# The first MLP's expanding product, by Strassen's scheme, with weights streamed from a scratch in DRAM

## The chip, the cores and the metric

One Trainium2 chip, of which this kernel uses one core. The time is device microseconds of one execution; the kernel before took 1018.35 us (median of two runs, 1016.62 to 1020.07). Engines are named as the profile names them: PE (TensorE, with PEld for its weight loads), DVE (VectorE), ACT (ScalarE), POOL (GpSimd) and SP (SyncE, which here only issues DMAs). Each runs its own list of instructions in order and waits for the others through semaphores.

## The reference, cut to what matters

```python
def _moe_ref(x, w_ch1, w_ch2):          # x: (4, 768, 512), the attention's output
    X = np.fft.fft(np.fft.fft(x, axis=1), axis=2)
    u = x + np.real(X)                  # "mix" is the second term
    un = (u - mean(u)) / np.sqrt(var(u) + 1e-06)
    ch = np.maximum(un @ w_ch1, 0.0) @ w_ch2      # 512 -> 2048 -> 512: the first MLP
    return u + ch
```

Ahead of it stands a windowed attention (8 heads of 64), behind it a second block (`_moe2_ref`): 512 -> 1024 with relu, a convolution of three taps along the sequence, a sigmoid gate, 1024 -> 512. All in float32.

## The kernel before, in words

**Precision.** The large products run in the one-pass float32 format of PE (`fp32r`). Each operand is kept as a high part, which is that rounding of it, and a low part, which is the rest; a product is three matmuls: low by high, high by low, high by high, added up in one PSUM bank.

**Three stages.** (1) `attention_and_fourier` handles the four batches of 768 tokens and leaves `mix` (the Fourier part) in a DRAM scratch. The order of its steps on each engine is written out by hand in the table `ORDER`: on PE the words `seq`, `dim` and `mix` are the two Fourier products and the turning of their result, on ACT `bh` and `mk` round or copy the results of `seq` and `mix`, on DVE `bl` and `cm` make the low parts and the combinations. Words `mlp0`, `mlp1`, ... in the last batch call the first steps of the next stage (`first_tensor`, `first_scalar`, ...), so that the two stages overlap. (2) `channel_mlp` is the first MLP. (3) `gated_conv` is the second block.

**The first MLP.** It works on half batches of 384 tokens (8 of them, g), and on 16 tiles of 128 hidden channels (m). For each pair (g, m), `expand` (L807) makes 384 tokens by 128 hidden channels from 4 chunks of 128 inputs: 12 matmuls of 384 columns. ACT (L722) takes relu and rounds (`h_hi`), DVE (L783) makes the low part (`h_lo`), and `contract` (L822) multiplies it with the second weight: 9 matmuls of 512 columns into three PSUM banks that add up over all 16 m. `expand` of m+1 stands before `contract` of m, so PE has work while ACT and DVE prepare h. In between DVE adds `mix` to u (L738), takes the statistics (L742, L747), normalises the next half (L771), PE turns it (L796, 4 transposes for 128 tokens) and ACT and DVE split it (L716, L777).

**Weights.** All 16 tiles of both weights stay in SBUF, 128x1024 numbers each: SP loads a tile (L686, three buffers, 512 KB), ACT rounds it (L708), DVE makes the low part (L729). This happens once, in the first half batch. `mix_in` for three tiles of tokens comes in one DMA of 768 KB (L679).

## Time and profile before

| | |
|---|---|
| median of two runs | 1018.35 us |
| the profiled execution | 1019.49 us, of which the span of the trace is 1017.4 us |
| granted PE clock, mean | 0.988 |
| busy: PE, DVE, ACT, POOL | 983.8, 433.2, 296.5, 175.3 us |
| matmuls | 6360 |
| first MLP's steady stretch | about 205 to 741 us |
| second block | 741 to 1017 us |

Busy times are sums over one engine; PE's matmuls overlap in the trace (a matmul's end is modelled), so what a matmul costs is read from the distance between starts, not from its own duration. A clock of 1.00 is 2.4 GHz and 0.50 is 1.2 GHz.

### The profile page before, as it was taken

To read this page: it belongs to the slowest core of one execution; us is meant where nothing else is said; L and a number is where in the kernel's file an instruction comes from. 1 tells how busy PE (TensorE), PEld (TensorE's weight loads), DVE (VectorE), ACT (ScalarE), POOL (GpSimd) and SP (SyncE) were. 2 spreads that over 40 slices of the span, in tenths; PEclk is the share of its full clock that TensorE was granted. 3 is DMA by queue.
4 is the path that set the end of the run, shared out by engine and by line. 5 is a ranking of instruction groups with operands and counts; after the bars stand their busy time and mean duration, and the time that the engine had idled before them with its cause. 6 is when DMAs were issued, how large, how long until landed. Compare 5 with 4: busy or idle time off the path is not lost.

```text
span 1017.4 us, 15409 instructions
## 1 busy us (share of the span) xinstructions
PE 983.8 (97%) x6360; PEld 885.5 (87%) x6360; DVE 433.2 (43%) x670; ACT 296.5 (29%) x535; POOL 175.3 (17%) x167
## 2 busy tenths in 40 slices
PE   4998997999999999999999999999999999999998
...
GB/s 337 397 220 312 310 155 229 203 146 43 93 1 1 93 1 36 58 1 93 0 0 93 0 31 62 1 129 91 42 93 1 65 60 1 124 0 41 21 1 63
DMA packets 41401, 92.73 MB, mean 91 GB/s; under 512 B 6912, under 2 KB 7040, under 8 KB 41088
## 3 DMA queue, kind: packets, MB, share of 16 engines
...
q0 software_dynamic: 576, 3.55, 0.9%
q8 instruction: 42, 0.69, 0.3%
...
## 4 chain that ended last, share of the span: by engine, by line
PE 92%; DMA 3%; SPq 1%; DVE 1%; issue 1%; POOL 1%; ACT 1%; ACTq 0%; POOLq 0%
PE ps L807 26%; PE ps L822 26%; PE ps L1171 13%; PE ps L1181 13%; PE ps L542 7%; DMA k_win<-in_k 3%; PE ps L506 2%; PE ps L533 2%; PE ps L1154 1%; PE ps L796 1%; PE ps L516 1%; SPq L249 1%; PE ps L598 1%; SPq L259 0%; SPq L245 0%
## 5 line engine op out<-in xcount | busy, mean ns | idle before, releaser
L807 PE MATMUL ps<-un_hi,w 128*128 128x384 f32 x1024 | 285.8, 339 | 1.6 <-ACT mix_sb L401 1.6
L822 PE MATMUL ps<-w,h_hi 128*128 128x512 f32 x768 | 241.0, 395 | 0.0
L807 PEld LDWEIGHTS ps<-un_hi,w 128*128 128x128 f32 x1024 | 187.2, 188 | 6.2 <-ACT mix_sb L401 1.8
L783 DVE SCALAR_TENSOR_TENSOR h_lo<-ps,h_hi 128x384 fp32r<-128x384 f32 x128 | 71.2, 556 | 280.1 <-ACT h_hi L722 280.1
L722 ACT ACTIVATE h_hi<-ps 128x384 fp32r<-128x384 f32 x128 | 62.9, 492 | 375.6 <-PE ps L807 375.6
L807 PE MATMUL ps<-un_lo,w 128*128 128x384 f32 x512 | 171.8, 336 | 0.0
L822 PEld LDWEIGHTS ps<-w,h_hi 128*128 128x128 f32 x768 | 144.0, 187 | 27.6
L822 PE MATMUL ps<-w,h_lo 128*128 128x512 f32 x384 | 149.4, 389 | 0.9 <-DVE h_lo L783 0.9
L1171 PE MATMUL ps<-y_hi,v 128*128 128x384 f32 x512 | 130.7, 334 | 0.8 <-issue 0.8
L1181 PE MATMUL ps<-v,g_hi 128*128 128x512 f32 x384 | 118.8, 391 | 0.0
L1136 DVE SCALAR_TENSOR_TENSOR conv<-h_pad,taps,conv 128x768 f32<-128x768 f32 x64 | 100.5, 1570 | 2.3
L1237 POOL TENSOR_TENSOR g_lo<-conv,g_hi 128x768 fp32r<-128x768 f32 x32 | 68.7, 2153 | 186.8 <-ACT g_hi L1105 186.8
L807 PEld LDWEIGHTS ps<-un_lo,w 128*128 128x128 f32 x512 | 96.2, 188 | 4.2
L1231 POOL MEMSET h_pad<- 128x6 f32 x1 | 0.1, 108 | 575.3 <-PE ps L822 575.3
L1171 PEld LDWEIGHTS ps<-y_hi,v 128*128 128x128 f32 x512 | 92.4, 188 | 1.3 <-issue 1.2
L1171 PE MATMUL ps<-y_lo,v 128*128 128x384 f32 x256 | 85.5, 334 | 0.0
L1181 PEld LDWEIGHTS ps<-v,g_hi 128*128 128x128 f32 x384 | 72.2, 188 | 14.8
L822 PEld LDWEIGHTS ps<-w,h_lo 128*128 128x128 f32 x384 | 72.2, 188 | 12.7 <-DVE h_lo L783 1.2
L1181 PE MATMUL ps<-v,g_lo 128*128 128x512 f32 x192 | 76.5, 398 | 0.0
L1171 PEld LDWEIGHTS ps<-y_lo,v 128*128 128x128 f32 x256 | 48.1, 188 | 0.1
L1124 DVE TENSOR_TENSOR y_lo<-ps,y_hi 128x512 fp32r<-128x512 f32 x24 | 16.6, 692 | 69.0 <-ACT y_hi L1086 69.0
L506 PE MATMUL ps<-k_win,q_sb 128*32 128x128 f32 x768 | 30.2, 305 | 14.5 <-DMA k_win<-in_k 14.5
...
## 6 DMA issues: line engine op xcount, KB each, us to landing
...
k_win<-in_k SPq DMA_DIRECT2D x48, 256.0 KB, 5.2
...
q_sb<-in_q SPq DMA_DIRECT2D x24, 256.0 KB, 4.7
mix_scratch<-mix_sb ACTq DMA_DIRECT2D x24, 256.0 KB, 6.2
u_sb<-x_scratch SPq DMA_DIRECT2D x8, 768.0 KB, 4.6
mix_in<-mix_scratch SPq DMA_DIRECT2D x8, 768.0 KB, 6.2
y_scratch<-u_sb SPq DMA_DIRECT2D x8, 768.0 KB, 3.6
```

Of the source, the lines that this page charges most:

```text
L506: last = nc.tensor.matmul(out, q_sb[:, n % NB, a, toks], k_win[:, n % NB, :, a, c, :], start=True, stop=True)
L533: last = nc.tensor.matmul(out, p_sb[:, t % 2, a, toks], v_win[:, n % NB, :, c, a, :], start=True, stop=True)
L542: last = nc.tensor.matmul(out, lhs, rhs, start=(n == 0), stop=(n == 3 * len(terms) - 1))
L722: nc.scalar.activation(h_hi[:, m % 2, :], ps[:, BH + m % 2, 0:HALF], ACT.Relu).then_inc(h_hi_ready, 1)
L783: nc.vector.scalar_tensor_tensor(out=h_lo[:, m % 2, :], in0=ps[:, BH + m % 2, 0:HALF], scalar=0.0, in1=h_hi[:, m % 2, :].bitcast(F32), op0 ...
L807: last = nc.tensor.matmul(ps[:, BH + m % 2, 0:HALF], w[:, cols], x[:, par, c, :], start=(k == 0), stop=(k == 3 * ND - 1))
L822: last = nc.tensor.matmul(ps[:, BACC[s], :], h[:, m % 2, cols], w, start=(m == 0 and j == 0), stop=(m == M1T - 1 and j == 2))
L1124: nc.vector.tensor_tensor(y_lo[:, :, cols], ps[:, BT, :].rearrange("p (c n) -> p c n", c=ND), y_hi[:, :, cols].bitcast(F32), ALU.subtract) ...
L1136: nc.vector.scalar_tensor_tensor(out=c, in0=h[:, j:S + j], scalar=taps[:, m, j:j + 1], in1=c, op0=ALU.mult, op1=ALU.add).then_inc(tap_done ...
L1171: last = nc.tensor.matmul(ps[:, BH[m % 2] + half, 0:HALF], w[:, cols], y[:, c, toks], start=(k == 0), stop=(k == 3 * ND - 1))
L1181: last = nc.tensor.matmul(ps[:, BACC[t], :], g[:, m, cols], w, start=(m == 0 and j == 0), stop=(m == M2T - 1 and j == 2))
L1237: nc.gpsimd.tensor_tensor(g_lo[:, m, :], conv[:, m % 3, :], g_hi[:, m, :].bitcast(F32), ALU.subtract).then_inc(g_lo_ready, 1)
```

## The change

The first MLP's `expand` takes a whole batch at once (768 tokens as two halves of 384), and a pair of hidden tiles (256 channels), as a product of 2 by 2 blocks: inputs 256 + 256, channels 128 + 128, tokens 384 + 384. Strassen's scheme (in Winograd's form) computes it with 7 products of blocks in place of 8, and 7 additions on the results; both operands need 4 sums of blocks each. There are 8 pairs for a batch (`PAIRS`) and 32 in all.

- **PE.** A pair is 7 products of 6 matmuls of 384 columns, each product in a PSUM bank of its own. Four pairs are expanded one after the other, and then their 8 hidden tiles are contracted for all 768 tokens into 6 banks (a group g, two for each batch): 18 matmuls of 512 columns for a tile.
- **ACT, DVE.** The results of a pair are added up in SBUF (`keep_first`, `combine`, `complete`: one copy on ACT, 7 additions on DVE), and relu and low part are then taken from SBUF, four times for a pair. After each group DVE adds the six accumulators to u (`add_up`).
- **Operands.** `upper`, `lower`, `upper_sums` and `lower_sums` make the 4 blocks and the 4 sums of the tokens (128x1024 numbers are rounded for 128 columns of the sums); POOL makes the 4 sums of a pair's weight blocks (`sums`, 128x256 numbers each), ACT and DVE round 128x7x256 numbers for a pair (`weights1`).
- **Weights.** They no longer fit in SBUF: 3 buffers for pairs (14,336 bytes a partition) and 4 for tiles of the second weight. In the first batch SP loads them raw, and stores high and low parts to a scratch in DRAM; from the second batch on POOL loads these from there (`stream_w1`, `stream_w2`).
- **Loads of mix** come one tile of tokens at a time through two buffers, each waiting for an addition on DVE (`load_mix`).
- **Order.** The words `mlpN` in the table stand for other steps and at other places; the loops over batches are written out. The second block differs in where its weights lie and when they are loaded.

```diff
+PAIRS, GROUP = 8, 8
...
+        "mix2.1 mix2.2 mix2.3 mix2.4 mix2.5 seq3.0 seq3.1 seq3.2 seq3.3 mlp0 seq3.4 seq3.5 mlp1 dim3.0 mlp2 "
+        "seq3.6 seq3.7 mlp3 dim3.1 mix3.0 mix3.1 mix3.2 mix3.3 mix3.4 mix3.5 mlp4 "
...
+        "mirror2.1 mk2.0 mk2.1 split3.5 mk2.2 mk2.3 mk2.4 mk2.5 bh3.0 mlp0 bh3.1 bh3.2 mlp1 mlp2 bh3.3 bh3.4 "
+        "mlp3 mlp4 bh3.5 mlp5 mlp6 mlp7 qs3.0 bh3.6 mirror3.0 bh3.7 mlp10 qs3.1 mirror3.1 mk3.0 mk3.1 mk3.2 "
+        "mk3.3 mk3.4 mk3.5 mlp8 mlp11 mlp9 "
...
+        "mlp0 mlp1 bl3.0 mlp2 mlp3 bl3.1 bl3.2 mlp4 mlp5 bl3.3 bl3.4 mlp6 mlp7 mlp8 bl3.5 mlp9 mlp10 mlp11 "
+        "mlp12 cm3.0 bl3.6 bl3.7 mlp15 cm3.1 mlp13 mlp16 mlp14 "
...
+        "lower3.3 fold3.5 lower3.4 lower3.5 mlp0 mlp1 mlp2 "
...
+    PRODUCTS = ((A11, B11), (S2, T2), (A12, B21), (S1, T1), (S3, T3), (S4, B22), (A22, T4))
+    P1, P6, P2, P5, P7, P3, P4 = range(7)
...
+    def load_mix(eng, b, s):
+        n = b * TILES + s
+        if n >= 2:
+            eng.wait_ge(u_ready, n - 1)
+        eng.dma_start(mix_in[:, s % 2], mix_dram[b, s]).then_inc(ld_mix[s % 2], 16)
+    def load_raw1(sp, n):
+        if n >= 3:
+            sp.wait_ge(product_done, 7 * (n - 2))
+            sp.wait_ge(st_w1[n % 3], 16 * (n // 3))
+        sp.dma_start(w1_raw[n % 3][:, A11:A12 + 1:A12 - A11, 1], w[2 * n][:, 0].rearrange("p (k c) -> p k c", k=2)
+                     ).then_inc(ld_raw1[n % 3], 16)
+        sp.dma_start(w1_raw[n % 3][:, S1:A22 + 1:A22 - S1, 1], w[2 * n + 1][:, 0].rearrange("p (k c) -> p k c", k=2)
+                     ).then_inc(ld_raw1[n % 3], 16)
...
+    def load_raw2(sp, j):
+        if j >= 4:
+            await_contracted(sp, j - 4)
+            sp.wait_ge(st_w2[j % 4], 16 * (j // 4))
+        sp.dma_start(w2_raw[j % 4][:, 1], w[j][:, 1]).then_inc(ld_raw2[j % 4], 16)
...
+    def store_w2(sp, j):
+        sp.wait_ge(w2_ready, j + 1)
+        sp.dma_start(w2_dram[j], raw(w2[j % 4][:])).then_inc(st_w2[j % 4], 16)
+    def stream_w1(pool, n):
+        pool.wait_ge(product_done, 7 * (n - 2))
+        if n < 2 * PAIRS:
+            pool.wait_ge(st_w1[(n - PAIRS) % 3], 16 * ((n - PAIRS) // 3 + 1))
+            pool.wait_ge(st_w1[n % 3], 16 * len([m for m in range(PAIRS) if m % 3 == n % 3]))
+        pool.dma_start(w1[n % 3][:], w1_dram[n % PAIRS]).then_inc(ld_w1[n % 3], 16)
...
+        sp.wait_ge(core.folded, 3 * TILES)
+        for i in range(FOLDS):
+            sp.wait_ge(core.st_x[i], 16 * (B - 1))
+        load_u(sp, 0)
...
+        for s in range(2):
+            load_mix(sp, 0, s)
...
+        load_raw1(sp, 0)
+        for s in range(2, TILES):
+            load_mix(sp, 0, s)
+        sp.wait_ge(core.seq_done, 8 * B)
+        for n in (1, 2):
+            load_raw1(sp, n)
...
+            nc.gpsimd.tensor_tensor(part(S3), part(A11), part(S1), ALU.subtract).then_inc(s_added, 1)
+            pool.wait_ge(s_added, 3 * n + 1)
+            nc.gpsimd.tensor_tensor(part(S1), part(S1), part(A22), ALU.add).then_inc(s_added, 1)
+            pool.wait_ge(s_added, 3 * n + 2)
+            nc.gpsimd.tensor_tensor(part(S2), part(S1), part(A11), ALU.subtract).then_inc(s_added, 1)
+            pool.wait_ge(s_added, 3 * n + 3)
+            nc.gpsimd.tensor_tensor(part(S4), part(A12), part(S2), ALU.subtract).then_inc(s_ready, 1)
...
+        def weights1(n):
+            act.wait_ge(s_ready, n + 1)
+            nc.scalar.activation(w1[n % 3][:, :, 0], w1_raw[n % 3][:, :, 1], ACT.Copy).then_inc(w1_hi_ready, 1)
...
+            for m, half, sums in ((2 * n, 0, 2), (2 * n, 1, 5), (2 * n + 1, 0, 6), (2 * n + 1, 1, 7)):
+                act.wait_ge(summed, 7 * n + sums)
+                nc.scalar.activation(hidden(m, half, 0), raw_hidden(m, half), ACT.Relu).then_inc(relu_done, 1)
...
+        def weights1(n):
+            dve.wait_ge(w1_hi_ready, n + 1)
+            nc.vector.tensor_tensor(w1[n % 3][:, :, 1], w1_raw[n % 3][:, :, 1], raw(w1[n % 3][:, :, 0]), ALU.subtract
+                                    ).then_inc(w1_ready, 1)
...
+        def plus(n, out, a, i):
+            dve.wait_ge(product_done, 7 * n + i + 1)
+            nc.vector.tensor_tensor(out, a, result(n, i), ALU.add).then_inc(summed, 1)
...
+        def combine(n):
+            c11, c12, c21, c22 = (raw_hidden(2 * n + r, half) for r in range(2) for half in range(2))
+            dve.wait_ge(copied, n + 1)
+            plus(n, c21, c12, P6)
+            plus(n, c11, c12, P2)
+            dve.wait_ge(summed, 7 * n + 2)
+            plus(n, c12, c21, P5)
+            plus(n, c22, c21, P7)
+            low_part(n, 2 * n, 0, 1)
...
+            c11, c12, c21, c22 = (raw_hidden(2 * n + r, half) for r in range(2) for half in range(2))
+            dve.wait_ge(summed, 7 * n + 4)
+            plus(n, c12, c12, P3)
+            plus(n, c21, c22, P4)
+            dve.wait_ge(summed, 7 * n + 6)
+            plus(n, c22, c22, P5)
+            low_part(n, 2 * n, 1, 2)
+            low_part(n, 2 * n + 1, 0, 3)
+            low_part(n, 2 * n + 1, 1, 4)
...
-        def expand(m, par):
...
-            for c in range(ND):
-                cols = slice(c * P, (c + 1) * P)
-                for w, x in ((w1_lo, un_hi), (w1_hi, un_lo), (w1_hi, un_hi)):
-                    last = nc.tensor.matmul(ps[:, BH + m % 2, 0:HALF], w[:, cols], x[:, par, c, :],
...
+        def expand(n):
...
+            if n < PAIRS:
+                pe.wait_ge(w1_ready, n + 1)
+            else:
+                pe.wait_ge(ld_w1[n % 3], streamed(n))
+            for i, (weight, tokens) in enumerate(PRODUCTS):
...
+                    elif i == P5:
+                        pe.wait_ge(summed, 7 * n)
...
+                for c in range(2):
+                    w_hi, w_lo = (w1[n % 3][:, weight, j, c * P:(c + 1) * P] for j in range(2))
+                    t_hi, t_lo = x_hi[:, tokens, c, :], x_lo[:, tokens, c, :]
+                    for a, b in ((w_lo, t_hi), (w_hi, t_lo), (w_hi, t_hi)):
+                        last = nc.tensor.matmul(result(n, i), a, b, start=(k == 0), stop=(k == 5))
+                        k += 1
+                last.then_inc(product_done, 1)
...
+            j, n = g * GROUP + m, 4 * g + m // 2
+            if j < M1T:
+                pe.wait_ge(w2_ready, j + 1)
...
+            for t in range(TILES):
...
+                        pe.wait_ge(summed, 7 * (4 * g + 3) + t)
+                    elif t == P5:
+                        pe.wait_ge(summed, 7 * (4 * g + 4))
...
+                for i, (part, weight) in enumerate(((1, 0), (0, 1), (0, 0))):
+                    last = nc.tensor.matmul(ps[:, t, :], h[:, m, part, cols], w2[j % 4][:, weight],
...
+        if k == 0:
...
+        elif k < 7:
+            (upper if k % 2 else upper_sums)(0, (k - 1) // 2)
+        elif k < 10:
+            weights1(k - 7)
+        else:
+            keep_first(k - 10)
+            rectify(k - 10)
...
+        if k < 2:
+            for s in range(3 * k, 3 * k + 3):
+                add(0, s)
+            for s in range(3 * k, 3 * k + 3):
+                stats(0, s)
+            if k == 1:
+                variance(0)
+        elif k == 2:
             inverse_root(0)
...
+        elif k in (3, 5, 8):
+            normalise(0, (3, 5, 8).index(k))
+        elif k in (4, 7, 10):
+            lower(0, (4, 7, 10).index(k))
+        elif k in (6, 9, 11):
+            lower_sums(0, (6, 9, 11).index(k))
+        elif k < 15:
+            weights1(k - 12)
+        else:
+            combine(k - 15)
+            complete(k - 15)
...
+        if k < 3:
+            turn(0, k)
+        else:
+            expand(k - 3)
...
+            for g in range(2 * B):
+                b, second = divmod(g, 2)
+                for p in range(4):
+                    n = 4 * g + p
+                    if n < PAIRS:
+                        store_w1(sp, n)
+                    if n + 3 < PAIRS:
+                        load_raw1(sp, n + 3)
+                    if g == 0 and p >= 2:
+                        for j in (2 * p - 4, 2 * p - 3):
+                            store_w2(sp, j)
...
+                if not second and b + 1 < B:
+                    load_u(sp, b + 1)
+                    for s in range(2):
+                        load_mix(sp, b + 1, s)
...
+                for m in range(GROUP):
+                    j = g * GROUP + m + 4
+                    if 4 < j <= M1T:
+                        store_w2(sp, j - 1)
+                    if j < M1T:
+                        load_raw2(sp, j)
+                    if not second and b + 1 < B and 1 <= m <= 4:
+                        load_mix(sp, b + 1, m + 1)
...
+            for g in range(1, 2 * B):
+                for p in range(4):
+                    if PAIRS <= 4 * g + p + 3 < B * PAIRS:
+                        stream_w1(pool, 4 * g + p + 3)
+                for m in range(GROUP):
+                    if M1T <= g * GROUP + m + 4 < B * M1T:
+                        stream_w2(pool, g * GROUP + m + 4)
...
+            for g in range(2 * B):
+                b, second = divmod(g, 2)
+                for p in range(4):
+                    n = 4 * g + p
+                    if n >= 2:
+                        combine(n)
+                        if 3 <= n + 1 < PAIRS and n + 1 not in (5, 6):
+                            weights1(n + 1)
+                        complete(n)
...
+                for m in range(GROUP):
+                    j = g * GROUP + m + 3
+                    if 4 <= j < M1T:
+                        weights2(j)
+                    if g == 0 and m in (0, 3):
+                        weights1(5 + m // 3)
+                    if not second and b + 1 < B and m < TILES:
+                        add(b + 1, m)
+                        stats(b + 1, m)
...
+                for t in range(TILES):
+                    add_up(g, t)
...
+            for g in range(2 * B):
+                b, second = divmod(g, 2)
+                for p in range(4):
+                    if 4 * g + p >= 2:
+                        expand(4 * g + p)
+                for m in range(GROUP):
                     contract(g, m)
...
+                    if second and b + 1 < B and m in (0, 2, 4):
+                        turn(b + 1, m // 2)
...
+        sp.wait_ge(core.product_done, 7 * B * PAIRS)
...
-            pe.wait_ge(core.y_ready, 2 * B * SUBS)
+            pe.wait_ge(core.y_ready, (2 * B - 1) * TILES + 4)
```

**What the order shows, ACT, end of the Fourier stage.** L401 to L409 copy `mix` (the words `mk3.*`) and L393 stores it; L813 rounds a pair's weights, L843 and L848 are `keep_first` and `rectify`. In the kernel before a tile's rounding (L708) stands among the `bh` steps; after it, on ACT:

```order
L409 ACTIVATE mix_sb<-ps 128x2
L393 DMA mix_scratch<-mix_sb 128x512
L813 ACTIVATE w_1_64<-w_1_raw 128x7x256
L843 ACTIVATE h_raw<-ps 128x384
L848 ACTIVATE h<-h_raw 128x384 x4
L813 ACTIVATE w_2_62<-w_2_raw 128x7x256
```

The second pair's weights are rounded behind the last copy of `mix`, and the third pair's behind the relus of the second.

**DVE, the first steps of the MLP.** Before (u and `mix` added, statistics, then the first `b_lo` of the last batch, L465):

```order
L738 TENSOR_TENSOR u_sb<-u_sb,mix_in 128x512 x3
L742 BN_STATS bn<-u_sb 128x6 x3
L747 BN_AGGR mv<-bn 128x2 x3
L749 TENSOR_SCALAR root<-mv 128x3
L465 TENSOR_TENSOR b_lo<-ps,b_hi 128x386
```

and of the change (the same `b_lo` is L473):

```order
L871 BN_STATS bn<-u_51 128x6 x3
L867 TENSOR_TENSOR u_51<-u_51,mix_in 128x512 x3
L871 BN_STATS bn<-u_51 128x6 x3
L876 BN_AGGR mv<-bn 128x2 x6
L878 TENSOR_SCALAR root<-mv 128x6
L473 TENSOR_TENSOR b_lo<-ps,b_hi 128x386
```

Six tiles of tokens instead of three now stand ahead of `b_lo`, and further down the rounding of the first pair (L855) stands ahead of the combination `cm3.0` (L483, L484):

```order
L928 TENSOR_TENSOR x_lo<-x_lo_raw,x_hi 128x8x128
L855 TENSOR_TENSOR w_0_60<-w_0_raw,w_0_60 128x7x256
L483 TENSOR_TENSOR m_all<-ps,q_sin 128x385
L484 TENSOR_TENSOR m_all<-ps,q_sin 128x385
L473 TENSOR_TENSOR b_lo<-ps,b_hi 128x386 x2
L935 TENSOR_TENSOR h_raw<-h_raw,ps 128x384 x4
L939 SCALAR_TENSOR_TENSOR h<-h_raw,h 128x384
```

**SP, the first contraction.** `w_0_raw` to `w_3_raw` are here the four buffers of the second weight, `w_scratch` the DRAM scratch:

```order
L738 DMA w_0_raw<-in_moe_w 128x512 [waits st_w2_0,contracted]
L746 DMA w_scratch<-w_0_68 128x1024 [waits w2_ready]
L738 DMA w_1_raw<-in_moe_w 128x512 [waits st_w2_1,contracted]
L721 DMA mix_in<-mix_scratch 128x512 [waits u_ready]
L746 DMA w_scratch<-w_1_70 128x1024 [waits w2_ready]
L738 DMA w_2_raw<-in_moe_w 128x512 [waits st_w2_2,contracted]
```

Each raw load of a tile stands behind the store of the tile before it, which waits until ACT and DVE have rounded that one.

## Rows read from the trace of the kernel before

**Rows 1.** The page, part 2: PE busy in tenths, 40 slices.
```profile
PE   4998997999999999999999999999999999999998
```
**Rows 2.** PE's timeline, steady MLP; start us, us, engine, line, form.
```profile
651.12 0.33 PE L807 MATMUL ps<-un_hi,w 128*128 128x384 f32 x1
...
653.22 0.39 PE L822 MATMUL ps<-w,h_lo 128*128 128x512 f32 x1
...
655.30 0.60 PE L796 MATMUL ps<-ident_sb,un 128*128 128x128 f32 x4
```
**Rows 3.** The page, part 5: busy, mean ns | idle before, releaser.
```profile
L807 PE MATMUL ps<-un_hi,w 128*128 128x384 f32 x1024 | 285.8, 339 | 1.6 <-ACT mix_sb L401 1.6
...
L783 DVE SCALAR_TENSOR_TENSOR h_lo<-ps,h_hi 128x384 fp32r<-128x384 f32 x128 | 71.2, 556 | 280.1 <-ACT h_hi L722 280.1
L722 ACT ACTIVATE h_hi<-ps 128x384 fp32r<-128x384 f32 x128 | 62.9, 492 | 375.6 <-PE ps L807 375.6
```
**Rows 4.** Windows: length, PE PEld DVE ACT POOL, PEclk, DMA share, GB/s.
```profile
165.00:741.00 576.00, 572.10 (x2934) 519.21 (x2934) 190.80 (x361) 118.90 (x231) 0.40 (x2) 1.00 0.17 58
...
40.00:45.00 5.00, 5.00 (x56) 4.52 (x56) 2.27 (x5) 2.60 (x5) 4.92 (x7) 1.00 1.04 410
```
**Rows 5.** PE's timeline, the last batch's first Fourier products.
```profile
165.17 0.66 PE L542 MATMUL ps<-seq_hi,z_lo 128*128 128x386 f32 x1 [0.83 <-ACT mix_sb L406]
...
168.20 0.44 PE L542 MATMUL ps<-seq_hi,z_lo 128*128 128x386 f32 x1
...
171.45 0.34 PE L542 MATMUL ps<-seq_hi,z_lo 128*128 128x386 f32 x1
```
**Rows 6.** DVE's timeline, the MLP's first steps.
```profile
163.48 2.97 DVE L738 TENSOR_TENSOR u_sb<-u_sb,mix_in 128x512 f32<-128x512 f32 x3 [5.16 <-DMA mix_in<-mix_scratch]
166.37 1.87 DVE L742 BATCH_NORM_STATS2 bn<-u_sb 128x6 f32<-128x512 f32 x3
...
168.62 0.17 DVE L749 TENSOR_SCALAR root<-mv 128x3 f32<-128x3 f32 x1
```
**Rows 7.** DMA issues: KB each, median us to landing.
```profile
mix_in<-mix_scratch SPq DMA_DIRECT2D x8, 768.0 KB, 6.2
...
out<-o_sb SPq DMA_DIRECT2D x24, 256.0 KB, 2.0
```
**Rows 8.** The line of the tile w_raw: landings of its 512 KB loads.
```profile
DMA to landing us min/median/max: 3.2/3.7/8.2
```
**Rows 9.** Groups by form: busy us, mean ns | idle before.
```profile
L1142 DVE TENSOR_TENSOR conv<-h_pad,conv 128x768 f32<-128x768 f32 x32 | 30.3, 948 | 0.2
...
L729 DVE TENSOR_TENSOR w<-w_raw,w 128x1024 fp32r<-128x1024 f32 x16 | 19.5, 1218 | 11.7 <-ACT w L708 11.7
...
L310 POOL TENSOR_TENSOR z_raw<-sums 128x256 f32<-128x256 f32 x24 | 17.5, 731 | 1.9
...
L708 ACT ACTIVATE w<-w_raw 128x1024 fp32r<-128x1024 f32 x16 | 16.8, 1052 | 0.5 <-ACT mix_sb L401 0.5
...
L777 DVE TENSOR_TENSOR un_lo<-ps,un_hi 128x512 fp32r<-128x512 f32 x24 | 16.6, 692 | 43.4 <-ACT un_hi L716 43.4
...
L357 ACT ACTIVATE z_hi<-z_raw 128x512 fp32r<-128x512 f32 x24 | 15.1, 628 | 13.6 <-POOL z_raw L311 10.9 <-ACT mix_sb L401 1.2 <-ACT mix_sb L396 0.9
...
L716 ACT ACTIVATE un_hi<-ps 128x512 fp32r<-128x512 f32 x24 | 14.4, 598 | 42.5 <-PE ps L796 42.5
```
**Rows 10.** ACT's timeline, copies of mix.
```profile
195.09 0.39 ACT L393 ACTIVATE mix_sb<-ps 128x256 f32<-128x256 f32 x1 [0.47 <-PE ps L598]
...
196.29 0.39 ACT L393 ACTIVATE mix_sb<-ps 128x256 f32<-128x256 f32 x1 [0.47 <-ACT mix_sb L396]
```
**Rows 11.** DVE's timeline, second block: first without, then beside POOL's work.
```profile
747.42 2.07 DVE L1136 SCALAR_TENSOR_TENSOR conv<-h_pad,taps,conv 128x768 f32<-128x768 f32 x2
...
760.59 3.55 DVE L1136 SCALAR_TENSOR_TENSOR conv<-h_pad,taps,conv 128x768 f32<-128x768 f32 x2
```

More of the change, by code:

```diff
@@ new lines, in raw, with streamed, turn_bank, hidden @@
+    def raw(t):
+        return t.bitcast(F32)
+    def streamed(n):
+        return 16 * len([m for m in range(PAIRS, n + 1) if m % 3 == n % 3])
+    def turn_bank(b, r):
+        return (2 if b == 0 else 6) + r
+    def hidden(m, half, part):
+        return h[:, m % GROUP, part, half * HALF:(half + 1) * HALF]
+    def raw_hidden(m, half):
+        return h_raw[:, m % GROUP, 1, half * HALF:(half + 1) * HALF]
+    def bank(n, i):
+        return i % 5 if n < 2 else i
+    def result(n, i):
+        return ps[:, bank(n, i), 0:HALF]
@@ L920, in _ @@
+        @block.gpsimd
+        def _(pool):
+            sums = on_gpsimd(pool)
+            for n in range(3, PAIRS):
+                sums(n)
+            for g in range(1, 2 * B):
[5 more added lines that the diff above has]
+                        stream_w2(pool, g * GROUP + m + 4)
         @block.scalar
```

641 lines of the change are left out of this document (314 added, 327 removed), and 8 rows, old and new, of the table ORDER.

## The prediction

> **What bounds the kernel now.** I read the busy shares first: PE is busy in nearly every slice of the MLP [rows 1], so what a matmul costs decides. Its own duration (339 ns, [rows 3]) overlaps with its neighbour's and can't be used. The timeline can: from 651.12 to 653.22 us stand the 12 matmuls of one `expand`, from there to 655.30 the 9 of one `contract` [rows 2]. That is 0.175 us for a matmul of 384 columns and 0.231 us for one of 512. DVE and ACT wait for PE in this stage (280 and 376 us of idle time before their h steps, [rows 3]), DMA is nearly idle, and PE lost only 576.0 - 572.1 = 3.9 us between 165 and 741 us [rows 4]. So fewer matmuls give their whole price, as long as nothing else makes PE wait. Everything up to 165 us and the second block I take as unchanged.
>
> **What is removed.** For a pair of hidden tiles and a batch, 48 matmuls of 384 columns become 42: 6 x 32 pairs = 192, at 0.175 us **33.6 us**. The 1152 matmuls of `contract` and the 96 turnings stay. The Trainium skill (TensorE: Matmul & The Clock Gate, "Back-to-back issue gap") gives N/2.4 + 2.5 ns, 162.5 ns here; by that the gain would be 31.2 us. The row decides.
>
> **Steady state after.** A pair takes PE 42 x 0.175 = 7.34 us. DVE has 7 additions from PSUM and 4 low parts from SBUF. An addition is like L783, 0.56 us [rows 3]. The low part now reads SBUF twice: two of L1136 on 768 numbers took 2.07 us [rows 11], a number costs (1218 - 948)/256 = 1.055 ns [rows 9], so 384 numbers take 1.03 - 0.41 = 0.62 us. Together 6.4 us, under 7.34. ACT has one copy and four relus of 0.5 us [rows 3]. A group is 4 x 7.34 + 8 x 4.15 = 62.6 us, in which 4 x 1.84 + 8 x 0.52 = 11.5 MB come from the scratch, 185 GB/s where 410 were moved [rows 4]. One block of 1.84 MB needs 4.5 us by that rate and about 2 us to start, and has two pairs' time, 14.7 us. So from the second batch on I cost the streaming and the sums at nothing; their cover is the 0.9 us a pair by which PE is longer than DVE.
>
> **What is added: the start.** The first batch pays for the rounding and for steps put in front of others. Prices: rounding a pair's 1792 numbers takes DVE 1.218 + 768 x 1.055 ns = 2.03 us, and ACT 1.052 + 768 x (1052 - 628)/512 ns = 1.69 us [rows 9]. POOL's four sums of 256 numbers take 4 x 0.73 = 2.9 us [rows 9]. Splitting 128 columns of tokens: ACT 0.6 + 3 x 0.27 = 1.4 us, DVE 1.8 us for the four sums and 1.0 us for two low parts, from 0.69 us for 512 numbers and 0.42 for 256 [rows 9]; ACT and DVE 1.0 and 1.2 us for 1024 numbers of the sums; normalising two tiles 1.0, a turning and its signal 1.0. A load of 256 KB lands in 2.0 us at the least [rows 7], and in less than the 3.7 us (3.2 at best) of 512 KB [rows 8]. I take 2.6 alone and 3.2 right behind a store of 512 KB.
>
> Walking the orders with these, PE waits:
> - a. **`seq3.3`, 6.9 us.** It needs the first `b_lo`, which now stands behind six tiles' additions and statistics. Before, three tiles came by one DMA and the variance was done at 168.8 [rows 6]. Now the third to sixth tile are each asked for only after an addition. First addition 164 (POOL's work slows it, as the 2.97 us for three show, [rows 6]); third 168; statistics 1.87; fourth 171; its buffer's load lands 173.9; last addition 174.6; statistics, variance 177.8; `b_lo` 178.3. PE arrives at 171.4 [rows 5].
> - b. **turning 1 and `dim3.0`, 8.2 us.** In line on DVE and ACT: turn 1.0, split 1.4 + 2.8, normalise 1.0, the same again, `b_lo` 0.5, 12.9 us; PE has 4.8 us of its own there.
> - c. **`seq3.7`, 7.7 us.** `dim3.0` 3.3, turn 1.0, split 1.4 + 1.8, sums 1.0, rounding of pair 0 1.7 + 2.0, `cm3.0` 1.0, 13.2 us; PE has 5.7.
> - d. **`mix3`, 3.9 us:** 1.8 behind pair 0's additions, 2.1 because ACT needs 1.20 us for a copy [rows 10].
> - e. **pair 1, 6.9 us:** three copies of `mix` are left, then 1.7 + 2.0.
> - f. **pair 2, 5.4 us:** its rounding stands behind pair 1's last additions and relu (1.7), then 1.7 + 2.0.
> - g. **pair 3, the first `contract` and pair 7, 1.2 us each:** 2.0 us of rounding stand between a pair's additions.
> - h. **pair 4, 11.6 us.** In the first contraction a raw tile is asked for only once the one before is rounded and its store issued: 0.3 + 3.2 + ACT 0.6 + DVE 0.65 + 0.4 = 5.2 us, where PE needs 4.15 us for a tile. Seven tiles stand ahead of DVE's `add_up`, without which PE may not reuse the banks; the chain also starts 2 us late, behind the next batch's loads of u, and pair 6's rounding lies in it.
> - i. **turnings of the later batches, 4.3 us** together.
>
> Sum 58.5 us. After a gap PE is slow too: from 165.17 to 168.20 nine matmuls took 3.03 us, the next nine to 171.45 two times 1.6 [rows 5], as if the clock were 1.2 GHz for 3 us. I charge 1.45 us for each of b, c, e, f and h, 7.2 us.
>
> DVE's work from two SBUF operands collides with POOL's sums: two L1136 took 3.55 us in place of 2.07 beside POOL [rows 11]. The Trainium skill (SBUF — State Buffer, "Who interferes with whom") makes this a lock: whoever starts first holds the shared ports for its whole instruction. By that a rounding waits for one sum at most, 0.7 us; were the ports shared by time, its 2.0 us would become about 3.4. POOL is rarely at work when DVE rounds, so I add nothing and leave 0 to 5 us to the range.
>
> **Sum.** 1019.5 (the profiled execution) - 33.6 - 3.9 (the old waits, counted anew) + 58.5 + 7.2 = 1047.7; the median lies 1.1 under the profiled execution, so **1046 us**.
>
> **Rivals.** About 2% (20 us) is what a measurement tells from no change.
> - *As summed* (60%): slower, 1034 to 1060. The waits a to f rest on the written order and on durations of rows; landings of 2.0 or 3.7 us move a and h by -10 to +8.
> - *The second weight keeps pace* (25%), the case on the other side: if a load lands in 2.1 us or less, h's period is 4.1 us, PE's own. Then h and its slow clock go, 13 us: 1033, not slower by the 2%. For it: 2.0 us for 256 KB [rows 7]. Against: that is a store, alone on its queue, and here a store of 512 KB goes ahead.
> - *DVE becomes the bound* (11%): 6.4 us leave 0.9 a pair. Each addition waits for a product or for its forerunner; with 0.15 us more for each of the 11, or one lock of 1.5 us a pair from POOL's DMAs, a pair takes 8.1 us, and 28 pairs 0.8 us more each: 1068.
> - *The gain stands* (4%): DVE and ACT run so far ahead that a to h are the old waits: 1018.4 - 33.6 = 985. Only a misread order would give it.
> - That the change doesn't save the matmuls is excluded: its list holds 1344 of 384 columns against 1536.
>
> Faster by over 2%: 3%. Within 2%: the second case and the low end of the first, 30%. Slower: 67%. The range for 8 in 10 is 1030 to 1066, which takes in the second case and nearly reaches the third.
>
> **What would show it.** The new profile should have PE's slices lower between 170 and 310 us only, full ones after; gaps before the first `b_lo`'s reader, `cm3.0`'s reader, pairs 1, 2 and 4, of 5 to 12 us, their releasers DVE; the start of the second block 25 to 30 us later than 741. A gap before pair 4 under 3 us means the second case. Waits of PE for DVE's additions or for a streamed block in each later group mean the third. I am wrong altogether if the MLP's first contraction starts before 240 us.

## The result and the profile after

The changed kernel took 1058.06 us (median of two runs, 1055.83 and 1060.29), the kernel before 1018.35: a ratio of 1.039, 95% interval 1.0269 to 1.0511. In a later set of runs on one chip (e11 below) it was 1060.38 against 1017.0, ratio 1.041, 1.0384 to 1.0436. So it is slower by 4%, at the upper end of the range forecast (1030 to 1066). The profiled execution took 1055.83 us, span 1054.0.

The page of the changed kernel, part 2, busy share in 40 slices (of 26.35 us each), answers to [rows 1]:

```profile
PE   5999986567859989999999999999999999999998
...
PEclk9899997678988989999999999999999999999999
```

The 7th to 12th slice, 158 to 316 us, are low, and the clock with them; the 15th has an 8; from the 16th on every slice is full, as before. What the slices hold is in the waits, TensorE's alone, from 160 to 800 us (line waiting, what it waited for: sum in us, times, longest):

```profile
PE ps L1017 <- DVE w L855: 15.1, 4, 7.3
PE ps L550 <- DVE b_lo L473: 13.1, 2, 7.4
PE ps L1017 <- DVE u L966: 12.1, 1, 12.1
PE ps L979 <- DVE un L902: 7.9, 5, 3.8
PE ps L550 <- DVE m_all L484: 7.4, 1, 7.4
PE ps L1041 <- DVE w L860: 4.6, 4, 2.1
PE ps L606 <- DVE m_all L484: 2.0, 1, 2.0
PE ps L1041 <- DVE h_raw L935: 1.1, 1, 1.1
```

They add up to 63.3 us in 19 waits, all on VectorE's results. What the clock does behind a wait stands in the timeline of TensorE, here at pair 1 and pair 2 (columns as in [rows 2]; a bracket gives the wait before the instruction and what ended it):

```profile
233.20 0.69 PE L1017 MATMUL ps<-x_hi,w 128*128 128x384 f32 x1 [7.26 <-DVE w L855]
233.69 0.53 PE L1017 MATMUL ps<-x_lo,w 128*128 128x384 f32 x1
234.01 0.84 PE L1017 MATMUL ps<-x_hi,w 128*128 128x384 f32 x2
...
238.49 0.40 PE L1017 MATMUL ps<-x_lo,w 128*128 128x384 f32 x1
238.72 0.52 PE L1017 MATMUL ps<-x_hi,w 128*128 128x384 f32 x2
...
242.95 0.34 PE L1017 MATMUL ps<-x_hi,w 128*128 128x384 f32 x1
249.29 0.69 PE L1017 MATMUL ps<-x_hi,w 128*128 128x384 f32 x1 [6.00 <-DVE w L855]
```

Behind the wait a matmul follows the other by 0.32 us, from 238.7 us on by 0.176: some 16 matmuls lost 0.145 us each. The granted clock is 1.2 GHz in the first part and 2.4 in the second.

The steady part is as forecast. Two windows (columns as in [rows 4]), 100 us with most of a group, and one pair of the third batch:

```profile
520.00:620.00 100.00, 99.48 (x517) 92.27 (x516) 63.92 (x126) 20.16 (x41) 9.53 (x19) 1.00 0.69 241
...
542.34:549.72 7.38, 7.38 (x44) 7.38 (x43) 5.67 (x12) 2.48 (x5) 0.53 (x1) 1.00 0.76 279
```

A pair takes TensorE 7.38 us (42 matmuls by 0.1757; the sum had 7.34 instead of the old 8.40), VectorE 5.67.

**One stretch to compare by.** The attention part in front has waits for transfers that differ from run to run. So kernels are compared below by S: the time from the last weight load of the attention's scores (L514) to the first weight load of the second block's products (L1388), each read from one profiled execution. For the changed kernel these are the last number of the first row and the first of the second:

```profile
L514 PEld LDWEIGHTS ps<-k_win,q_sb x768: 105/110/178, 7.0 to 136.3; 128*32 128x32 f32 x192
...
L1388 PEld LDWEIGHTS ps<-y_hi,v x512: 187/188/188, 777.9 to 1017.7; 128*128 128x128 f32 x171
```

S is 641.6 us; before it was 741.3 - 142.7 = 598.6. The change costs 43.0 us there, while the span grew by 36.6: in this profile the attention part was 6.4 us shorter, and e11 shows that this is scatter.

| kernel | time, us | ratio to before (95%) | S, us |
|---|---|---|---|
| before | 1018.35 | 1 | 598.6 |
| changed | 1058.06 | 1.039 (1.027 to 1.051) | 641.6 |
| e11, the same again | 1060.38 | 1.041 (1.038 to 1.044) | 640.6 |
| e1, load ahead of store | 1038.78 | 1.021 (1.018 to 1.024) | 622.3 |
| e2, pairs 1 and 2 rounded early | 1053.21 | 1.035 (1.031 to 1.039) | 636.9 |
| e5, e2 and early store of pair 0 | 1047.89 | 1.029 (1.027 to 1.032) | 629.8 |
| e3, waits filled | 1048.22 | 1.029 (1.026 to 1.033) | 633.0 |
| e4, four cures | 1027.38 | 1.009 (1.006 to 1.011) | 608.5 |
| e6, eight cures | 1015.26 | 0.998 (0.996 to 0.9995) | 596.8 |
| e9, e6 with two places mended | 1010.42 | 0.992 (0.990 to 0.995) | 589.5 |
| e10, e9 with one wait filled | 1009.32 | 0.992 (0.990 to 0.995) | 591.6 |
| e7, two low parts twice | 1063.07 | 1.045 (1.042 to 1.047) | 642.4 |
| e8, four low parts twice | 1064.85 | 1.046 (1.043 to 1.048) | 648.5 |

The kernel before took 1017.5 beside e1 to e4, 1018.2 beside e5 to e8, 1017.0 beside e9 to e11. The letters a to i of the waits are those of the prediction.

### The profile page after: what moved, and what is told of

It is laid out like the page before. It is cut to its first block, busy times and chain, and to the rows that moved or that the text cites. A ratio compares the mean times of both kernels' runs of the same rounds, so it can differ in the third digit from the quotient of the medians.

```text
span 1054.0 us, 15426 instructions
## 1 busy us (share of the span) xinstructions
PE 964.6 (92%) x6168; PEld 866.9 (82%) x6168; DVE 597.1 (57%) x962; ACT 335.2 (32%) x607; POOL 238.6 (23%) x271
## 4 chain that ended last, share of the span: by engine, by line
PE 80%; DMA 9%; DVE 6%; ACT 2%; SPq 1%; issue 1%; POOL 0%; ACTq 0%; DVEq 0%; POOLq 0%
PE ps L1017 22%; PE ps L1041 20%; PE ps L1388 13%; PE ps L1398 12%; PE ps L550 6%; DMA w_raw<-in_moe_w 4%; PE ps L541 2%; DMA k_win<-in_k 2%; PE ps L514 2%; DMA mix_in<-mix_scratch 1%; DMA v_win<-in_v 1%; PE ps L979 1%; DVE h L939 1%; PE ps L1371 1%; PE ps L524 1%
## 5 line engine op out<-in xcount | busy, mean ns | idle before, releaser
L1041 PE MATMUL ps<-w,h 128*128 128x512 f32 x1152 | 270.3, 394 | 5.6 <-DVE w L860 4.6
L1017 PE MATMUL ps<-x_hi,w 128*128 128x384 f32 x896 | 239.0, 346 | 27.2 <-DVE w L855 15.1
L1041 PEld LDWEIGHTS ps<-w,h 128*128 128x128 f32 x1152 | 216.3, 189 | 51.7 <-DVE w L860 6.3
L1017 PEld LDWEIGHTS ps<-x_hi,w 128*128 128x128 f32 x896 | 167.9, 194 | 29.1 <-DVE w L855 16.3
L935 DVE TENSOR_TENSOR h_raw<-h_raw,ps 128x384 f32<-128x384 f32 x224 | 123.2, 553 | 74.5 <-PE ps L1017 68.3
L1017 PE MATMUL ps<-x_lo,w 128*128 128x384 f32 x448 | 154.1, 344 | 0.0
L1388 PE MATMUL ps<-y_hi,v 128*128 128x384 f32 x512 | 130.6, 334 | 0.0
L848 ACT ACTIVATE h<-h_raw 128x384 fp32r<-128x384 f32 x128 | 67.1, 526 | 164.2 <-DVE h_raw L935 162.0
L1388 PEld LDWEIGHTS ps<-y_hi,v 128*128 128x128 f32 x512 | 92.5, 188 | 0.2
L1017 PEld LDWEIGHTS ps<-x_lo,w 128*128 128x128 f32 x448 | 86.8, 194 | 0.2
L1388 PE MATMUL ps<-y_lo,v 128*128 128x384 f32 x256 | 85.6, 334 | 0.0
L939 DVE SCALAR_TENSOR_TENSOR h<-h_raw,h 128x384 fp32r<-128x384 f32 x128 | 68.4, 575 | 0.0
L966 DVE TENSOR_TENSOR u<-ps,u 128x512 f32<-128x512 f32 x48 | 31.9, 689 | 63.4 <-PE ps L1041 63.4
L843 ACT ACTIVATE h_raw<-ps 128x384 f32<-128x384 f32 x32 | 15.3, 478 | 139.5 <-PE ps L1017 139.5
L550 PE MATMUL ps<-seq_hi,z_lo 128*128 128x386 f32 x96 | 37.5, 391 | 15.2 <-DVE m_all L484 7.4
```

What stands on the lines that cost most here:

```text
L550: last = nc.tensor.matmul(out, lhs, rhs, start=(n == 0), stop=(n == 3 * len(terms) - 1))
L848: nc.scalar.activation(hidden(m, half, 0), raw_hidden(m, half), ACT.Relu).then_inc(relu_done, 1)
L935: nc.vector.tensor_tensor(out, a, result(n, i), ALU.add).then_inc(summed, 1)
L939: nc.vector.scalar_tensor_tensor(out=hidden(m, half, 1), in0=raw_hidden(m, half), scalar=0.0, in1=raw(hidden(m, half, 0)), op0=ALU.max, op ...
L966: nc.vector.tensor_tensor(u_sb[b % 2][:, t, :], ps[:, t, :], u_sb[b % 2][:, t, :], ALU.add).then_inc(y_ready, 1)
L1017: last = nc.tensor.matmul(result(n, i), a, b, start=(k == 0), stop=(k == 5))
```

## The experiments

**e11: is the shorter attention part the change's?**

> The changed kernel once more, in ten runs beside the kernel before, for a narrower ratio. If the five microseconds by which the attention part was shorter in its profile (its last scores at 136.7 us against 143.1) belong to the change, this profile shows them again; if they are scatter of the transfers there, the last scores end anywhere from 136 to 144 us, as in e1 to e8, and the median is 1055 to 1062.

```profile
L514 PEld LDWEIGHTS ps<-k_win,q_sb x768: 106/110/178, 6.9 to 144.3; 128*32 128x32 f32 x192
...
L1388 PEld LDWEIGHTS ps<-y_hi,v x512: 186/188/188, 784.9 to 1024.6; 128*128 128x128 f32 x171
```

The last scores of the same kernel now begin at 144.3 us instead of 136.3, and S agrees to 1 us. In all runs they lie between 136.3 and 144.3. It is scatter, and S is the number to read. Single waits scatter too: in e11 the later turning waits 3.1 us instead of 3.8 and the longest wait of the turning of mix is 2.8 instead of 2.0, so differences of that size between two profiles say nothing.

**e1: the second weight's serial chain (wait h).** Only the order of SyncE's issues in the contraction:

```diff
+                    if j < M1T:
+                        load_raw2(sp, j)
                     if 4 < j <= M1T:
                         store_w2(sp, j - 1)
-                    if j < M1T:
-                        load_raw2(sp, j)
```

> Only the order of SyncE's issues in the contraction of the first batch is changed: a raw tile of the second weight is asked for before the store of the one ahead of it, not behind it. Theory 'serial chain' (landing, two roundings and the store's signal in line, 5.2 us a tile where TensorE needs 4.15): the load then waits only for a free buffer, four tiles ahead of its use, so the three waits in the first contraction (0.84, 0.75, 0.93 us), most of the 12.1 us before pair 4 and the 3.8 us before a turning at 379 us go, and with them 4.5 us of slow clock: 22 us less, 1036 us; about 1 us is left before pair 4. Rival 'traffic' (the loads land late because stores, x and the second weight share the queues, whoever asks first): landings become longer by as much as they are asked earlier, and the time stays within 5 us of 1058. Rival 'DVE is late anyway': pair 4 keeps a wait of 5 us or more for the additions, and the time is 1045 or more.

First the chain in the changed kernel; the timelines of SyncE, ScalarE and VectorE in the first contraction:

```profile
291.82 0.32 SPq L746 DMA_DIRECT2D w_scratch<-w  x1
292.24 0.38 SPq L738 DMA_DIRECT2D w_raw<-in_moe_w  x1
...
295.56 0.63 ACT L817 ACTIVATE w<-w_raw 128x512 fp32r<-128x512 f32 x1 [4.50 <-DMA w_raw<-in_moe_w]
...
296.23 0.69 DVE L860 TENSOR_TENSOR w<-w_raw,w 128x512 fp32r<-128x512 f32 x1 [3.10 <-ACT w L817]
...
296.95 0.32 SPq L746 DMA_DIRECT2D w_scratch<-w  x1
...
317.32 0.69 DVE L860 TENSOR_TENSOR w<-w_raw,w 128x512 fp32r<-128x512 f32 x1 [4.28 <-ACT w L817]
317.93 3.67 DVE L966 TENSOR_TENSOR u<-ps,u 128x512 f32<-128x512 f32 x6
```

Asked at 292.24, on ScalarE at 295.56 (3.3 us), rounded by 296.9, and only then the next store and load: 5.13 us from store to store. The whole period from store to store is 5.0 to 5.6 us in this contraction. VectorE comes to the six `add_up` (L966) at 317.9, though TensorE had ended at 306.7. Behind the edit, TensorE's waits on these two lines in e1:

```profile
PE ps L1041 <- DVE w L860: 2.1, 1, 2.1
PE ps L1017 <- DVE u L966: 2.0, 1, 2.0
```

4.1 us are left of 16.7, and the 3.8 us before a turning at 379 us, of the same chain, are gone. S fell by 19.3 us, and the time by as much, of the 22 forecast: the chain was the cause. The rival "traffic" wanted landings longer by as much as they are asked for earlier; the median landing of the 256 KB loads went from 3.5 to 3.8 us.

**e2 and e5: the place of a rounding in the list (waits e and f).** e2 moves the rounding of pairs 1 and 2 (ScalarE's step 10 has pair 1's between its relus):

```diff
-... bh3.7 mlp10 qs3.1 mirror3.1 mk3.0 ... mk3.5 mlp8 mlp11 mlp9
+... bh3.7 mlp10 qs3.1 mlp9 mirror3.1 mk3.0 ... mk3.5 mlp11
-... mlp15 cm3.1 mlp13 mlp16 mlp14
+... mlp15 cm3.1 mlp13 mlp14 mlp16
```

> Only the place of the rounding of pairs 1 and 2 is changed: ScalarE rounds pair 1 between the relus of pair 0 and pair 2 ahead of the Fourier mirror, VectorE both right behind the Fourier combination and ahead of pair 1's additions. Theory 'written order' (waits e and f are the place of these two steps in the lists, the data being there since 218 us): the 7.3 us before pair 1 and the 6.0 us before pair 2 go, and 4 us of slow clock with them: 17 us less, 1041 us, with up to 2 us given back because the copies of the mix stand behind a rounding. Rival 'shared ports' (rounding is late because GpSimd's sums run beside it): VectorE's 2.03 us for a rounding become 3 us or more and pair 2 still waits over 3 us. Rival 'passed on': pair 3 and the first contraction inherit the wait, and the time is above 1050.

Both waits are gone, but S fell by 4.7 us only, not 17. Of the three theories "passed on" was right, and the trace of e2 shows where to; SyncE, GpSimd, VectorE and TensorE in order of time:

```profile
232.11 0.46 SPq L742 DMA_DIRECT2D w_scratch<-w  x1
241.79 0.38 SPq L728 DMA_DIRECT2D w_raw<-in_moe_w  x1
...
245.82 0.72 POOL L800 TENSOR_TENSOR w_raw<-w_raw 128x256 f32<-128x256 f32 x1 [23.22 <-DMA w_raw<-in_moe_w]
...
251.59 2.02 DVE L855 TENSOR_TENSOR w<-w_raw,w 128x1792 fp32r<-128x1792 f32 x1
...
253.67 0.69 PE L1017 MATMUL ps<-x_hi,w 128*128 128x384 f32 x1 [9.61 <-DVE w L855]
```

Pair 3 takes pair 0's buffer. The store of pair 0 is issued at 232.1 and has to land (9.7 us) before raw pair 3 is asked for; with landing, sums and roundings TensorE has it 21.6 us after the store. In the changed kernel pair 1 and 2 wait so long that this is hidden. So e5 adds, in SyncE's list ahead of its wait for the turned mix:

```diff
         for n in (1, 2):
             load_raw1(sp, n)
+        store_w1(sp, 0)
+        load_raw1(sp, 3)
```

> The kernel of e2, and the store of the rounded pair 0 and the load of raw pair 3 are issued by SyncE ahead of its wait for the turned mix (pair 0 is rounded at 204 us, its store was issued at 227 to 228). Theory 'passed on to the buffer': in e2 pair 3 waited 9.6 us because it takes the buffer of pair 0, whose 1.8 MB store had to land first, and the load, GpSimd's four sums and two roundings (some 11 us) come behind it; with the store 12 us or more earlier this wait falls under 2 us, its slow clock goes, and the 17 us forecast for e2 are there: 1041 us. Rival 'traffic' (the load of raw pair 3 lands late for whatever reason): pair 3 keeps over 5 us and the time stays at 1050.

```profile
215.92 0.47 SPq L742 DMA_DIRECT2D w_scratch<-w  x1
...
224.65 0.37 SPq L728 DMA_DIRECT2D w_raw<-in_moe_w  x1
```

Pair 3 waits 0.95 us now, S is 629.8: 11.8 us less than the changed kernel, of 17. Part of the rest was passed on once more, to what had been just in time: the fifth tile of the second weight waits 4.4 us instead of 2.1, and the first contraction 2.1 instead of 1.1. The turning of mix (3.7 instead of 2.0) and a later turning (5.1 instead of 3.8) are longer too, of which some may be the scatter seen in e11.

**e3: the clock.** 221 matmuls that nobody reads, in six waits; for instance before pair 2:

```diff
+            if n in (1, 2, 4):
+                if n < 4:
+                    pe.wait_ge(summed, 7 * (n - 1) + 5)
+                for _ in range({1: 34, 2: 28, 4: 60}[n]):
+                    nc.tensor.matmul(ps[:, 7 if n == 4 else 0, 0:HALF], x_hi[:, 0, 0, 0:P], x_hi[:, 0, 0, :], ...)
```

> Nothing is moved; TensorE gets matmuls whose results nobody reads, in the six longest waits (36 before the fourth and the eighth Fourier product of the last batch, 27 before its first product over channels, 34, 28 and 60 before pairs 1, 2 and 4), somewhat shorter than the waits themselves. Theory 'clock': the slow stretches behind the waits (13.0 us in all behind these six) exist only because TensorE had been idle; the granted clock stays at 1.00 there, and 10 to 13 us go although no wait is cured: 1046 us. Rival 'the matmuls after a wait are slow for want of data' (first operands, semaphores): they stay slow, and the time stays at 1058 or rises by what the added matmuls overrun.

TensorE's timeline at pair 2, to be set beside the changed kernel's 249.29 above:

```profile
237.72 5.02 PE L998 MATMUL ps<-x_hi 128*128 128x384 f32 x28
...
243.87 0.44 PE L1032 MATMUL ps<-x_hi,w 128*128 128x384 f32 x1 [1.12 <-DVE w L864]
244.14 0.34 PE L1032 MATMUL ps<-x_lo,w 128*128 128x384 f32 x1
244.33 0.51 PE L1032 MATMUL ps<-x_hi,w 128*128 128x384 f32 x2
```

The rhythm is 0.176 us from the second matmul on. The window from 167 to 333 us, first of the changed kernel, then of e3:

```profile
167.00:333.00 166.00, 110.52 (x503) 100.29 (x504) 89.55 (x150) 49.15 (x93) 19.06 (x25) 0.81 0.46 165
```
```profile
167.00:333.00 166.00, 145.35 (x775) 134.39 (x774) 98.58 (x171) 52.88 (x99) 26.63 (x30) 0.99 0.51 186
```

The granted clock is 0.99 instead of 0.81. Behind the six waits 13.0 us had been lost to the slow clock, in e3 1.0. S fell by 8.6, some 3 us less than the 12 won on the clock: waits that no matmul filled were longer (the later turning 5.4 instead of 3.8, the second weight's tiles 5.3 instead of 4.6, the turning of mix 2.8 instead of 2.0, as in e11). Idle time, not want of data, slows the matmuls behind a wait.

**e4: do the waits add up?** e1 and e2 together; pair 0 rounded while the first tokens are added (`mlp7` ahead of `mlp0` on ScalarE, the low part ahead of the last addition on VectorE); and `bh3.5`, `bl3.5` ahead of the second splitting.

> The edits of e1 and e2 together, and two more: the rounding of pair 0 while the first tokens are added (ScalarE had been idle there for 9 us), no longer ahead of the Fourier combination, and the last Fourier rounding of the half batch ahead of the second splitting of tokens. Theory 'waits add up': e1 returns 22, e2 17, the wait before the eighth Fourier product falls from 7.5 to 3.8, the 5.7 before the product over channels to 2, and 2 to 3 us of slow clock: 49 us less, 1009 us, which is under the kernel before (1018). Rival 'the next one is just as late': each cure is partly passed on, half of the sum is left, 1033 us.

S fell by 33.1 us of 49. e2's part was passed to pair 3 (9.4 us) here too, which e5 had still to show. Of the two new cures one gave more than forecast (the wait for `b_lo` before the product over channels: 5.65 us became 0.3), the other less (7.4 became 5.05, forecast 3.8). The combination still stood behind the last splitting of tokens; e6 moves it ahead, and there this wait is gone.

**e6, e9, e10: a version that beats both.** e6 is e4 with e5's early store, `qs3.0` and `cm3.0` ahead of the last splitting, x and mix of batch 1 asked for during pair 2, and mix of four tiles loaded at once into `x_raw`, which is free until the first splitting.

> The kernel of e4 with four more cures: the store and load of e5; the Fourier combination ahead of the last splitting of tokens on ScalarE and VectorE; x and mix of the second batch asked for during pair 2 and not in front of the fifth tile of the second weight; mix of four tiles of the first batch loaded at once into memory of the token parts, not through two buffers one after the other. Theory 'waits add up': against e4 (1027) pair 3 gives 8 us and 1.7 of clock, the fifth tile of the second weight 4 and 1.7, the eighth Fourier product 2.5, the first Fourier rounding 3.5: 21 us, 1006 us, under the kernel before (1017.5) by over 1%. Rival 'the next one is just as late': half of it, 1017 us, no gain over the kernel before.

Forecast 1006, measured 1015.26; S 596.8. Pair 3's wait fell from 9.4 to 0.94 and the eighth product's went, while a new one of 2.5 us came before pair 0, for the split tokens. But the first Fourier wait stayed at 7.1 (pair 0's low part, 2.0 us, now stood in front of the last addition), and the fifth tile of the second weight waited 7.2. SyncE in e6:

```profile
246.86 1.01 SPq L746 DMA_DIRECT2D w_scratch<-w  x1
...
256.06 0.38 SPq L732 DMA_DIRECT2D w_raw<-in_moe_w  x1
...
258.04 2.24 SPq L742 DMA_DIRECT2D w_raw<-in_moe_w  x2
```

SyncE waits for the landing of the store of pair 3, issued at 246.86, and asks for raw pair 6 9.2 us later (the trace has 9.1 us for the landing); the load that TensorE needs next (258.04) is queued behind that wait. e9 puts it in front, `bl3.0` ahead of three statistics, and pair 0's low part behind `bl3.2`:

```diff
+                    if n == 3:
+                        load_raw2(sp, 4)
+                        load_raw1(sp, 6)
-... bl3.0 mlp2 mlp3 bl3.1 bl3.2 mlp4 mlp5 ...
+... bl3.0 mlp2 mlp3 bl3.1 bl3.2 mlp12 mlp4 mlp5 ...
```

> The kernel of e6 with two places mended. SyncE asks for the fifth tile of the second weight ahead of raw pair 6, whose wait for the 9 us landing of the store of pair 3 had stood in front of it; and VectorE rounds the first Fourier product ahead of the statistics of tiles 4 to 6, and pair 0 of the weights behind the second Fourier rounding instead of ahead of the last addition. Theory 'whatever stands in front in the list': the 7.2 us before the fifth tile's contraction fall under 1 us and take 2 us of clock with them, and the first Fourier wait falls from 7.1 to about 3 us: 12 us less than e6 (1015.3), 1003 us, 1.4% under the kernel before. Rival 'traffic': TensorE waits for the same landings elsewhere, and no more than 4 us are gained, 1011 us.

TensorE's longest waits in e9, 160 to 800 us:

```profile
PE ps L990 <- DVE un L913: 6.9, 7, 3.0
PE ps L606 <- ACT mix_sb L404: 4.1, 6, 1.4
PE ps L1028 <- DVE u L977: 3.3, 1, 3.3
PE ps L1028 <- DVE x_lo L939: 2.5, 1, 2.5
```

S is 589.5, 7.3 less than e6 and 9.1 less than before; the time is 1010.42 us, ratio 0.9924 to the kernel before. 12 us were forecast over e6, 4.8 measured in the median. So the seven products can win, by 0.8% (0.5 to 1.0), once the first batch is put in order. All waits of this window sum to 25.8 us.

> e9 with 14 unread matmuls before the fourth Fourier product of the last batch, 2.5 us in a wait of about 3. If idle time is what slows the clock there, 1 to 2 us less than e9; if not, the same as e9 within 1 us.

1009.32, the same ratio; S was 2 us longer. The forecast was 1 to 2 us less. The wait that was to be filled was 1.2 us in e9, not the 3 assumed, so 2.5 us of matmuls overran it and nothing was there to gain: inconclusive on the clock, which e3 had settled.

**e7 and e8: is VectorE near to being the bound?** From the second batch on, a low part is made again into spare memory:

```diff
+            if n >= PAIRS and i <= 2:      # e8: 4
+                nc.vector.scalar_tensor_tensor(out=spare[:, i - 1], in0=raw_hidden(m, half), scalar=0.0, ...)
```

> The changed kernel, and from the second batch on VectorE makes two low parts of a pair of tiles twice, the second time into memory nobody reads: 2 x 0.5 us more for a pair. Theory 'cover': TensorE's pair takes 7.4 us and VectorE's 6.2, so 1.0 us more is still covered: 1058 us, within 3 us. Rival 'VectorE is already the bound, or its steps stand in TensorE's way one by one': each of the 24 pairs becomes up to 1 us longer, 1070 us or more.

> As e7 with all four low parts twice: 4 x 0.5 us more for a pair. Theory 'cover': 8.2 us of VectorE against 7.4 of TensorE for a pair, so up to 0.8 us for each of 24 pairs, less what a group of four pairs can be behind before TensorE needs a bank: 8 to 20 us more, 1066 to 1078, with waits of TensorE for the additions in every group. If VectorE had over 2 us to spare a pair, the time stays at 1058; if it had none, 48 us are added.

e7: 1063.07, but S 642.4 against 641.6 and 640.6. Its median lies 2.7 us above that of e11; since S does not show it, the attention part is the likely place, but only one execution of e7 was profiled. e8: S 648.5, 7 us more, in the slowest of its four runs; its median is 4.5 us above that of e11, under the 8 to 20 forecast. TensorE's waits from 400 to 800 us, e7 and e8:

```profile
PE ps L984 <- DVE un L904: 2.0, 2, 1.0
```
```profile
PE ps L984 <- DVE un L904: 4.6, 2, 2.3
```

Neither shows a wait for an addition. Back to back a low part starts 0.47 us after the one before, so e8 adds 1.9 us, and 5.67 + 1.9 = 7.6 is just over the pair's 7.38. VectorE then enters the contraction late: from the second batch on the last low part of a group ends 2.7 us behind the contraction's first matmul in the changed kernel, 3.2 in e7, and 4.2 to 4.5 in e8. The turnings pay (12.1 us from 160 to 800 us, against 7.9), and behind one of them 1.6 us of slow clock. VectorE had some 1.7 us to spare for a pair.

## Why the prediction was right, and where its sizes were off

The direction, the mechanism and most of the steps came out; the time lies inside the range, 12 us above the point forecast. Span for span it had +28.2 us; measured was +36.6, and +43.0 over S. So the sum was 15 us short over S, and 6.4 of these don't show in the span by luck, because the attention part of that execution was shorter. The start of the second block came 36.6 us later, where the prediction's own sign was 25 to 30. Step by step, idle time of TensorE:

| step | forecast, us | changed kernel |
|---|---|---|
| a, first `b_lo` | 6.9 | 7.4 |
| b, turning 1 and `dim3.0` | 8.2 | 2.0 + 5.7 |
| c, `seq3.7` | 7.7 | 7.4 |
| d, mix3 | 3.9 | 2.0 |
| e, pair 1 | 6.9 | 7.3 |
| f, pair 2 | 5.4 | 6.0 |
| g, pair 3, first contraction, pair 7 | 3.6 | 0.9 + 1.1 + 0.9 |
| h, pair 4 and second weight | 11.6 | 12.1 + 4.6 |
| i, later turnings | 4.3 | 1.0 + 3.8 + 0.5 + 0.5 |
| sum | 58.5 | 63.2 |
| slow clock | 7.2 | 14.2 |
| matmuls | -33.6 | -33.6 |

The last two of the right column: 192 matmuls at the 0.175 us that the steady part confirms; and, over all matmuls of 384 columns and more, what each start was later than by the fast rhythm, less the same sum before. 63.2 less the 3.2 us of old waits, 14.2, and -33.6 make 40.6 of the 43.0; 2.4 us I can't place. Three small slips of the prediction's arithmetic change nothing: its own terms give 8.1 for b and 7.5 for c, and 1047.7 - 1.1 is 1046.6.

- **The saving, right.** 7.38 us a pair, and from 400 us on the clock is at 1.00 and TensorE waits 1.0 us in all before the second block. The formula that the prediction took from the Trainium skill (TensorE: Matmul & The Clock Gate, "Back-to-back issue gap") is by that section the gap of an isolated matmul, and for a stream with weight loads it has about 131 ns at 512 columns. The rows have 231 ns there and 175.7 at 384, so neither figure holds here and the row was rightly preferred.
- **Waits a to g, right** to 2 us each: they come from the written order, and order and durations of rows give them. e2 and e5 show that these sizes are no prices: curing e and f alone gave 4.7 us in e2, not 13.3 and their clock, and 11.8 with pair 0's store moved as well.
- **h, the mechanism right, the size 5 us short.** The tile's period was 5.0 to 5.6 us where I had 5.2, but I booked only what ends before pair 4, and left out the four waits inside the contraction. The case "the second weight keeps pace" is refuted: from the request to ScalarE's start went 3.3 us in the row shown, the shortest landing of a 256 KB raw load was 2.7, and it would have had to be 2.1. The 2.0 us of [rows 7] were a store's.
- **The slow clock, the term that was mis-sized**: 7.2 against 14.2. I charged five waits, and it followed seven; and I took 1.45 us from [rows 5], where the last wait had been 0.83 us long. Behind waits of 3.8 to 12.1 us 1.4 to 2.9 us are lost. The row was real but belonged to shorter waits.
- **VectorE as the bound** was sized too near: I added durations (6.4 us a pair) where neighbours overlap by some 0.08 us, the thing that I had corrected for TensorE and not for VectorE; a low part also took 0.55 us, not 0.62. The window has 5.67, and e7 and e8 agree.
- **SBUF's ports, right to add nothing.** In the changed kernel's first profile all eight roundings of the first weight took 2.01 to 2.03 us. In e11 one met a sum of GpSimd that had begun 0.26 us earlier; VectorE's and GpSimd's timelines:

```profile
253.63 2.54 DVE L855 TENSOR_TENSOR w<-w_raw,w 128x1792 fp32r<-128x1792 f32 x1
...
253.37 0.92 POOL L804 TENSOR_TENSOR w_raw<-w_raw 128x256 f32<-128x256 f32 x1
254.37 2.39 POOL L806 TENSOR_TENSOR w_raw<-w_raw 128x256 f32<-128x256 f32 x1
```

  The rounding took 0.52 us more, and the sum that came during it 2.39 us in place of the 0.73 of [rows 9]: it ends 0.59 us behind the rounding. Were the ports shared half and half while both are at work, the rounding would have taken some 3.2 us and that sum some 1.5 (an estimate from 2.02 and 0.73 and these starts). In e3 three of the eight roundings met sums, and none took over 2.57 us; one of them, and the sum that came during it:

```profile
241.25 2.57 DVE L864 TENSOR_TENSOR w<-w_raw,w 128x1792 fp32r<-128x1792 f32 x1 [0.78 <-ACT w L822]
...
242.01 2.39 POOL L813 TENSOR_TENSOR w_raw<-w_raw 128x256 f32<-128x256 f32 x1
```

  By the Trainium skill (SBUF — State Buffer, "Who interferes with whom") whoever starts first holds the ports for its whole instruction; the traces agree with their 2.54 to 2.57 and 2.39 us.
- What I took as unchanged up to 165 us scatters by 8 us from run to run.
